# Half of the first pair's RMS scaling moved to GpSimd, and a row in device memory laid out by partitions

## The reference

```python
# attention: batch 4, 8 heads, 576 positions, head size 64, causal window of 64
scores = where(0 <= i - j < 64, q @ k.T / 8, -1e9); attn = softmax(scores); x = attn @ v
x = x.reshape(2304, 512)                      # tokens x features
# first layer
xn = x / sqrt(mean(x * x, axis=-1) + 1e-6) * rms_g
x = (silu(xn @ w_gate) * (xn @ w_val)) @ w_out    # 512 -> 1536 -> 512
# second layer
x = relu(x @ w_in) ** 2 @ w_down                  # 512 -> 2048 -> 512
```

## Time and profile before

| what | value |
|---|---|
| median of 3 runs | 870.01 us (869.5 to 870.76) |
| profiled execution, its time | 869.6 us |
| profiled execution, span from first to last instruction | 867.8 us |
| mean granted clock of TensorE | 0.998 of full speed |
| TensorE busy | 851.2 us, 98% of the span |
| VectorE busy | 588.8 us, 68% |
| ScalarE busy | 477.2 us, 55% |
| GpSimd busy | 468.0 us, 54% |

### The profile page before, as it was taken

How to read it: one execution, slowest core, us unless ns; L and a number is a source line. 1 busy time by engine, 2 the same in 40 slices (tenths; PEclk the granted TensorE clock), 3 DMA queues, 4 the chain that set the end, 5 groups by cost and what they waited for, 6 DMA issues and landing times.

```text
span 867.8 us, 16812 instructions
## 1 busy us (share of the span) xinstructions
PE 851.2 (98%) x6390; PEld 839.5 (97%) x6390; DVE 588.8 (68%) x729; ACT 477.2 (55%) x1001; POOL 468.0 (54%) x471
## 2 busy tenths in 40 slices
PE   7898999999999999999999999999999999999998
PEld 6787999999999999999999999999999999999998
DVE  4668776468557558755557767678677777677982
ACT  6787566545565645555554455554455454555451
POOL 4656398493589665388857368222187212386100
PEclk9999999999999999999999999999999999999999
DMA  8773122322222232222222322256622266523587
GB/s 300 246 225 88 49 74 74 64 77 61 82 72 73 74 73 61 79 74 74 73 56 61 85 68 74 55 164 225 218 86 71 71 222 185 169 73 98 179 254 246
DMA packets 109871, 100.98 MB, mean 116 GB/s; under 512 B 8544, under 2 KB 87520, under 8 KB 109792
## 3 DMA queue, kind: packets, MB, share of 16 engines
q1 hardware_dynamic: 92544, 84.04, 32.8%
q10 hardware_dynamic: 17248, 15.87, 5.5%
HBM read 80.48 MB, written 19.40 MB: 115 GB/s over the span
## 4 chain that ended last, share of the span: by engine, by line
PE 91%; DVE 3%; issue 2%; ACT 2%; POOL 1%; DVEq 0%; POOLq 0%; ACTq 0%
PE banks L840 29%; PE banks L841 29%; PE banks L842 29%; ACT probs L1165 1%; PE banks L810 1%; DVE probsT L1498 1%; PE banks L751 1%; PE banks L824 1%; PE banks L784 1%; DVE acts L1438 0%; DVE banks L1478 0%; PE banks L759 0%; POOL h L689 0%; POOL d_lo L696 0%; DVE xc_lo L1629 0%
## 5 line engine op out<-in xcount | busy, mean ns | idle before, releaser
L840 PE MATMUL banks<-xc_hi,w_hi 128*128 128x384 f32 x844 | 282.5, 335 | 0.2 <-DVE xc_lo L1470 0.2
L842 PE MATMUL banks<-xc_hi,w_lo 128*128 128x384 f32 x844 | 281.9, 334 | 0.0
L841 PE MATMUL banks<-xc_lo,w_hi 128*128 128x384 f32 x844 | 281.9, 334 | 0.0
L840 PE MATMUL banks<-hs_hi,d_hi 128*128 128x384 f32 x544 | 182.3, 335 | 0.8 <-POOL d_lo L696 0.6
L842 PE MATMUL banks<-hs_hi,d_lo 128*128 128x384 f32 x544 | 181.7, 334 | 0.0
L841 PE MATMUL banks<-hs_lo,d_hi 128*128 128x384 f32 x544 | 181.7, 334 | 0.0
L840 PEld LDWEIGHTS banks<-xc_hi,w_hi 128*128 128x128 f32 x844 | 158.4, 188 | 0.6 <-DVE xc_lo L1470 0.4
L841 PEld LDWEIGHTS banks<-xc_lo,w_hi 128*128 128x128 f32 x844 | 158.4, 188 | 0.0
L842 PEld LDWEIGHTS banks<-xc_hi,w_lo 128*128 128x128 f32 x844 | 158.4, 188 | 0.0
L1414 DVE TENSOR_TENSOR w_lo<-w_raw,w_hi 128x1024 fp32r<-128x1024 f32 x58 | 75.6, 1303 | 82.1 <-ACT w_hi L1086 81.8
L578 POOL TENSOR_TENSOR w_raw<-w_raw 128x256 f32<-128x256 f32 x58 | 61.8, 1065 | 122.1 <-DVE d_lo L1584 52.2
(11 more groups left out here) (115 smaller groups left out, 1333.7 us busy)
## 6 DMA issues: line engine op xcount, KB each, us to landing
w_kept<-stash SPq DMA_DIRECT2D x56, 256.0 KB, 3.2
w_raw<-in_w_gate SPq DMA_DIRECT2D x36, 256.0 KB, 2.9
w_raw<-in_w_val SPq DMA_DIRECT2D x72, 128.0 KB, 2.9
d_raw<-in_w_out SPq DMA_DIRECT2D x36, 256.0 KB, 2.6
d_raw<-in_w_down SPq DMA_DIRECT2D x32, 256.0 KB, 2.9
v_sb<-in_v_rows SPq DMA_DIRECT2D x16, 384.0 KB, 4.3
w_raw<-in_w_in SPq DMA_DIRECT2D x24, 256.0 KB, 2.7
w_raw<-in_w_in SPq DMA_DIRECT2D x48, 128.0 KB, 2.6
```

Of the source, the lines that this page charges most:

```text
L840: pe.matmul(ps, w_h, v_h, start=first, stop=False, skip_group_check=joined)
L841: pe.matmul(ps, w_h, v_l, start=False, stop=False, skip_group_check=joined)
L842: return pe.matmul(ps, w_l, v_h, start=False, stop=last, skip_group_check=joined)
```

## The change

There are two parts.

1. The second half of the first pair is no longer scaled by VectorE. In slot 12 GpSimd multiplies its four blocks by the gain (`times_gain`, 128x384 by a per-partition number), behind its three small steps. In slot 16 ScalarE, behind `x_high(B21)`, waits for the spread roots and copies them from bank 5 to an SBUF tile `rb0` (the free half of a squares tile). GpSimd, behind its three small steps of slot 16, waits for that copy and multiplies blocks 0 and 1 by it (`times_root`), and behind those of slot 17 blocks 2 and 3. The readers of the second half wait for `half_normed` in place of `norm_done`, and the counts of `norm_done` shrink by KT. `x_high(B11)` now waits for two normalised blocks, not for four.
2. The row of inverse roots in device memory is written in the order of `rms` in SBUF: six neighbouring numbers for each partition, not one number every 128. The load stays as it is. `normalise` of pairs 1 and 2 reads `rb` with a stride of six numbers, so that the values meet their tokens.

```diff
+        rb0 = squares[0][3][:, 0:NT]
...
+        def by_block(t):
+            return t.rearrange("p (n t) -> p n t", n=TB)
...
+            def times_gain(k):
+                x = half_cols(0, k, 1)
+                nc.gpsimd.tensor_scalar(x, x, gain[:, k:k + 1], None, ALU.mult).then_inc(gained, 1)
+            def times_root(k):
+                x = half_cols(0, k, 1)
+                pool.wait_ge(gained, k + 1)
+                nc.gpsimd.tensor_tensor(x, x, rb0, ALU.mult).then_inc(half_normed, 1)
...
+                if g == 12:
+                    pool.wait_ge(gain_in, 16)
+                    pool.wait_ge(sq_pool, KT + 2)
+                    pool.wait_ge(sq_done, 2)
+                    for k in range(KT):
+                        times_gain(k)
...
+                if g in (16, 17):
+                    pool.wait_ge(rb_kept, 1)
+                    for k in (2 * (g - 16), 2 * (g - 16) + 1):
+                        times_root(k)
...
-                act.dma_start(rinv_rows[q, :].rearrange("(n p) -> p n", p=P), rms[:], allow_slow_non_contiguous=True).then_inc(rows_out, 16)
+                act.dma_start(rinv_rows[q, :].rearrange("(p n) -> p n", p=P), rms[:]).then_inc(rows_out, 16)
...
-                    if first_layer(r):
+                    if r == 0 and b in ("B12", "B22"):
+                        act.wait_ge(half_normed, n)
+                    elif first_layer(r):
...
-                    x_high(0, ("B11", "B21")[g - 15], KT)
+                    x_high(0, ("B11", "B21")[g - 15], 2 * (g - 14))
+                if g == 16:
+                    act.wait_ge(rb_first, 2)
+                    copy(rb0, bank[5][:, 0:NT], rb_kept)
                 if g in (17, 18):
-                    x_high(0, ("B12", "B22")[g - 17], 2 * KT)
+                    x_high(0, ("B12", "B22")[g - 17], 2 * (g - 16))
...
-                if g in (16, 17):
-                    if g == 16:
-                        x_low(0, "B11")
-                        dve.wait_ge(rb_first, 2)
-                    for k in (2 * (g - 16), 2 * (g - 16) + 1):
-                        normalise(half_cols(0, k, 1), k, bank[5][:, 0:NT])
+                if g == 16:
+                    x_low(0, "B11")
...
-                                normalise(pair_cols(q, f - 1), f - 1, rb[:])
+                                normalise(by_block(pair_cols(q, f - 1)), f - 1, rb[:].rearrange("p (t n) -> p n t", n=TB))
```

More of the change, by code:

```diff
@@ L279, in build @@
         rms_done, rinv_done, diag_done = sem("rms_done"), sem("rinv_done"), sem("diag_done")
-        rb_first = sem("rb_first")
+        rb_first, rb_kept, gained, half_normed = sem("rb_first"), sem("rb_kept"), sem("gained"), sem("half_normed")
         rows_out, rb_in, norm_done = sem("rows_out"), sem("rb_in"), sem("norm_done")
@@ L1328, in _ @@
                         if s == 2 and r > 0:
-                            act.wait_ge(norm_done, 2 * KT + KT * r)
+                            act.wait_ge(norm_done, KT + KT * r)
                             act.wait_ge(ms_mm, r + 1)
@@ L1353, in _ @@
                     if q < RUNS:
-                        normed = 2 * KT + KT * q
+                        normed = KT + KT * q
                         if f == 3 + 2 * (r in KEEPING):
@@ L1451, in x_sum @@
                         dve.wait_ge(h22_done, U0[r] - U0[PAIRS])
-                    if first_layer(r):
-                        dve.wait_ge(norm_done, 2 * KT + KT * r)
+                    if r == 0:
+                        dve.wait_ge(half_normed, KT)
+                    elif first_layer(r):
+                        dve.wait_ge(norm_done, KT + KT * r)
                     else:
```

## The result

The changed kernel takes 877.16 us, median of 4 runs (876.12 to 878.67), against 870.11 before on the same chip (869.5 to 870.76): ratio 1.0084, 95% interval 1.0066 to 1.0101, so 7.05 us slower. The forecast was 870.9 with a range up to 873.0. The profiled execution took 878.67 us, with a span of 876.8, against 869.6 and 867.8: 9.1 us. It is the slowest of the four, and the one with the lowest mean clock: 0.992, where the other three were granted 0.994 (877.76), 0.996 (876.56) and 0.998 (876.12).

What follows compares the result with a forecast made beforehand. TensorE, busy nearly all the span, was taken as the bound, so only its idle time counts. +1.4 (detour) +1.1 (clock) -1.6 (store) = +0.9 on the profiled 869.6: 870.5, or 870.9 against the median; range 869.6 to 873.0.

Steps and rivals of the forecast that it cites:

- I take 0.5 and cost 0: Down-projection, runs 0 and 1: the strided read adds 0.5 us to each scaling and costs the kernel nothing.
- Added d per chunk slips GpSimd d - 0.4, four times: nothing for TensorE up to d = 0.65: Down-projection: a scaling longer by d us delays GpSimd d - 0.4 in each of four chunks, harmless up to 0.65.
- Rival B: Down-projection chunks 1 to 4, runs 0 and 1: the strided read decides, 3.6 us on top, 874.5; chance 15%.
- the order on GpSimd's queue: Slot 17: root products ahead of GpSimd's small steps delay `probsT` and the value products, 75.61 to 77.43; net loss 1.40 us.
- the fall of the clock behind the hole: Attention stage: TensorE's hole grows from 1.6 to 3.46 us, its clock then likely halves; loss 1.1 us.
- part 1 as a whole: Attention stage, second half scaled on GpSimd: loss 1.4 us from the detour and 1.1 from TensorE's clock.
- Rival A: Attention stage: TensorE's clock stays up behind the hole; 1.4 - 1.6 = -0.2, 869.8 us; chance 18%.
- rival D: Attention stage: the GpSimd detour is hidden and VectorE's freed time counts; -2.9, 867.1 us; chance 8%.
- the gain products: GpSimd, slot 12: four products, up to 0.6 us each by the cast, 1.01 from above; cost 0 at either bound.
- cover ends: GpSimd, slot 12: the gain products stop being hidden if one takes over 1.05 us.
- the store: Row written by partitions: lands in 3 to 4.4 us, removing ScalarE's wait; gain 1.6 us in run 0, nothing in run 1.
- Rival C: End of run 0: the store's gain is absent because median executions seldom had the hole; +2.5, 872.5 us; chance 14%.

Runs made afterwards that it cites:

- stride_only: The kernel before, with only the read of the row made strided and the store left as it was: 874.55 us against 869.79, ratio 1.0057.
- row_copied: The whole change, but ScalarE copies the row once into token order and the scalings read the copy: 871.86 us against 869.77 for the kernel before, ratio 1.002.
- part2_only: The kernel before, with only the row stored by partitions and read with a stride: 873.25 us against 869.79, ratio 1.0048.
- hole_filled: Only the second half's scaling moved to GpSimd, and TensorE multiplies ones 24 times in the hole: 874.12 us against 869.94 for the kernel before, ratio 1.0049.
- roots_late: Only the second half's scaling moved to GpSimd, root products behind the small steps of slots 17 and 18: 869.56 us against 869.94 before, ratio 0.9996.
- part1_only: The kernel before, with only the second half's scaling moved to GpSimd, row store and read as before: 872.29 us against 869.79, ratio 1.0029.

## Why the prediction was wrong

**The step that failed is "I take 0.5 and cost 0"**, with the rule under it: "Added d per chunk slips GpSimd d - 0.4, four times: nothing for TensorE up to d = 0.65". It stands for the strided read, which cost 2.4 to 2.6 us in each of two runs. Rival B had the mechanism, the place (chunks 1 to 4, runs 0 and 1) and nearly the price: 3.6 us on top, against +4.8 for stride_only and 5.0 between row_copied and the changed kernel (7.05 - 2.1). It was given 15%, and the range left most of it out. Two things were mis-sized.
- The added duration d. Counted as the forecast counted, from the end of GpSimd's instruction to that of the scaling, the work is 0.81 with neighbours and 1.45 to 1.50 with the step of 24 bytes. So d is some 0.65, and not 0.5: the very border of the forecast's rule.
- The slip. By the rule d = 0.65 still costs nothing, so the rule is wrong by more than d. It let GpSimd slip the same 0.25 in each chunk, 1.0 in four, which the lead would cover. The first chunk does so: `d_lo` to `d_lo` is 4.29 in place of 4.16. The next ones take 5.48 and 6.08, a slip of 1.3 and 1.9. Once late, GpSimd no longer meets one VectorE instruction per chunk but several. In the 5.48 `hs_lo` holds both the first `d_lo` (2.01, not 1.55) and the second sum (1.34, not 0.74), and the scaling holds the first sum (2.13, not 1.46). In the 6.08 it meets two scalings, at 190.63 and 194.65. Its weight sums and `d_lo` are busy 261.8 us before, 269.3 in part2_only and 275.7 in stride_only: 0.9 to 1.7 us for each of the eight scalings, of which d itself is 0.65.

Of the two figures that the Trainium skill gives (Vector Engine (DVE) Microarchitecture Reference, 5.2 Measured stream behaviour on trn2), neither fits here. As estimates they made 0.5 or 1.1 us more for 768 columns; the step of 24 bytes added 0.65. A step of 8 bytes on one source cost the scaling nothing (2043 ns in the mean, 2047 with neighbours in row_copied), where 1.73 ns a column would have made 0.5.

**Right, by rows:** the order on GpSimd's queue, first root product to `probsT` to value products (forecast +1.82, measured 4.79 - 2.98 = 1.81); 0.97 for each root product while VectorE is idle (forecast 1.0), and of the later pair one held up by `x_low(B21)`: 1.72 and 0.99; the fall of the clock behind the hole, though 1.1 was too little (1.3 to 1.6 by hole_filled); part 1 as a whole (+2.5 against +2.5 in the medians and, up to the next value products, 2.7 in the traces). Rival A and rival D are refuted by the same rows. roots_late shows that D's idea, VectorE's freed time counting, is real as soon as the order permits: value products 1.92 behind the first plain ones, not 2.98. Most of it is lost again at the last value products.

**Right answer, wrong size:** the gain products, 1.25 us each and not 0.6, past the "cover ends" of 1.05 and past the upper bound of 1.01. The cost stayed at 0 net, since the 0.7 lost by slot 14 comes back before slot 16. The forecast's condition was too strict.

**Half right:** the store. Landing 3.2 us as forecast, and 1.6 gained in the profile; in the medians 0.6 (869.16 against 869.79) or, beside the strided read, 1.3 (873.25 against 874.55). Rival C's reason is seen in part1_only's run 0: with the old store landing in 10.1 us there is next to no hole (57.22). How often the executions behind the medians have it, no run shows.

**The sum:** part 1 +2.5 and part 2 +3.5 make 6.0, the whole change shows 7.05. About 1 us is left, and its cause stays open. The profile after has 1.55 us with half clock in slot 13 that no other kernel's profile shows, and a start 0.8 later. row_copied, with the same attention stage, kept its clock there (16.29 to the spread). The changed kernel's four executions were granted 0.992 to 0.998 in the mean and row_copied's twelve 0.994 to 0.998, and four are too few to say whether it loses the clock more often. The intervals of the three medians (1.1 to 1.6 us to either side) cover the difference too.

## What to carry to other kernels

Price a new access pattern for the engine beside it too: here the strided scalings grew by 0.4 us in the mean and GpSimd's instructions by 0.9 to 1.7 for each, and GpSimd was the one that TensorE waited for. Slack that is counted chunk by chunk holds only while the two engines keep step: past it, the late one meets more of the other's instructions, and the loss jumps. When work moves to another engine, its place in that engine's queue decides more than its duration: the same four products cost 2.5 us ahead of three small steps, and behind them nothing that the interval tells. And where one row of numbers is read by several large instructions, one reordering copy on an engine with time (1.64 us of ScalarE) keeps the cheap transfer and the cheap read.

## What the runs showed of the hardware

- A scaling of 128x768 on VectorE with its row in steps of 24 bytes takes 2.12 to 2.73 us beside GpSimd; in steps of 8 bytes, 2.04, as with neighbours. Beside the first, a GpSimd sum of 128x256, 0.74 alone, takes as much as 2.14 and `d_lo`, 1.28 alone, up to 2.67; beside the other two a sum takes 1.46.
- The two engines take turns in all 13 traces: the scaling ends 0.81 us (neighbours, or 8 bytes) or 1.45 to 1.50 (24 bytes) after the GpSimd instruction that was running when it started, and a weight sum beside it ends 0.6 after the scaling.
- GpSimd's product of 128x384 with one number per partition takes 1.25 us. That is more than its product of two whole tensors in the same kernel, 0.99 with VectorE idle and 1.72 beside `x_low(B21)`.
- 3 KB from SBUF to device memory land in 2.2 to 3.9 us as 128 pieces of 24 bytes (six traces) and in 9.4 to 11.6 as 768 of 4 (seven).
- Two executions whose windows agree within 0.07 us in every engine's busy time (52.6 to 56.5, TensorE 3.12 and 3.11 of 3.90) were granted 0.55 and 1.00 in the next 3.3 us. So what the engines did there does not decide it alone; the 3.5 us with almost nothing in them were followed by a fall in all four kernels that had them and left them empty.
